# Attention scores of two heads at once, in plain fp32, in place of a split query times a split key

## The chip, the cores and the metric

The kernel runs on one core of one Trainium2 chip. The metric is the device time of the whole program in microseconds (us); a run's time is that of one launch.

## What is computed

Causal attention over a window of 128 keys plus 4 sink keys, then a mixture of experts with greedy assignment, then a dense feed-forward layer. Only the first step of the attention, the scores, is touched by the change:

```python
B, H, S, D = q.shape                        # 2, 8, 768, 64
scale = 1.0 / np.sqrt(D)
scores = scale * np.matmul(q, k.transpose(0, 1, 3, 2))
...
scores = np.where(keep, scores, -1000000000.0)   # 4 sinks, 128 keys back
scores = scores - np.max(scores, axis=-1, keepdims=True)
a = np.exp(scores)
a = a / (np.sum(a, axis=-1, keepdims=True) + 1e-09)
return np.matmul(a, v).astype(np.float32)
```

Its result `x`, 1536 tokens by 512, goes through `_moe_ref` (8 experts, 192 tokens each, 512 to 1024 to 512) and `_moe2_ref` (512 to 2048 to 512).

## The kernel before

The attention works on blocks of 128 queries. There are 2 batches times 6 blocks, so 12 steps (`STEPS`), and each step has 8 heads. For one head and one step the scores are a tile of 128 queries by 260 keys: the block's own 128 keys, the 128 before them, and 4 sinks.

The work is a pipeline by hand. Every engine runs `attention_slot(s)` for s = 0, 1, 2, and so on, and one slot holds pieces of three steps: the scores, the row maximum and the exponential of step s (`front`), the transposes of the probabilities, the sink terms and half of the products with v of step s - 1 (`mid`), and the rest of those products and the turn back to token rows with the gate's logits of step s - 2 (`end`). Slots 0 and 1 have nothing older to work on, and slots 12 and 13 have no scores. The order inside an engine is that of the loop over `h` in its `attention_slot`; between engines there are only semaphores.

**Scores before.** TensorE's fast fp32r form rounds its operands, so each operand is split in a rounded part and what is left. Host code hands q and k over twice, in partitions 0 to 63 and again in 64 to 127. `q_hl` holds the rounded q in the upper half of the rows and the rest in the lower half; `k_hi` and `k_lo` are the rounded k and its rest, in both halves. Two fp32r matmuls over all 128 rows (L1199), `q_hl` times `k_hi` and `q_hl` times `k_lo`, add up to the full product of one head in one of three PSUM banks (`S_BANK`). The split is made by other engines: ScalarE rounds k (L334, `round_next_k`), GpSimd rounds q (L328), and subtracts to get `k_lo` (L346) and the lower half of `q_hl` (L339). For the first two steps ScalarE and VectorE do parts of it.

**Around it.** `head_max` on VectorE (L817) reads a bank, applies the mask, writes the negated scores and their minimum, and so frees the bank. ScalarE's L642 is the exponential. `turn_prob` on TensorE (L1217) transposes a head's 128 by 256 probabilities in two instructions; a pair of heads fills a PSUM bank, which VectorE (L857, three of four pairs) or ScalarE (L662, one of four) copies to `prob_t`. `turn_sinks` (L1226), `sink_values` (L1237), `values` (L1253) and `turn_and_gate` (L1274) are the other matmuls of a slot. `values` writes one head to PSUM rows 0 to 63 and the next to rows 64 to 127, each through 64 columns of the array. `keep_clock` (L1174) multiplies zeros where TensorE would have nothing to do, 19 times before the first scores.

**Queues.** The SP queue loads q and k of step t + 2 in pass t of its loop, behind waits on `qk_split`, then stores a finished x block, then loads v. After the attention, later code sorts out routing (VectorE, L906) and runs experts and the feed-forward layer (L1409, L1418, L1500, L1511).

Of the kernel before, what the change touches and what calls it, by code (L numbers as in the profile page):

```python
# [17 lines left out]
F32 = mybir.dt.float32  # L18
# [11 lines left out]
P = 128  # L30
CAP = N // E
QB = S // P
# [25 lines left out]
def program(nc, q_t, k_t, k_sink, v_rows, v_sink_d, wg_d, w1_d, w2_d, w_in_d, w_out_d, alpha_d, out, n_sink, window):  # L58
# [9 lines left out]
    with ctx:  # L68
# [42 lines left out]
        q_raw = [sb(f"q_raw{b}", [P, H, P], at=early) for b in range(2)]  # L111
        k_raw = [sb(f"k_raw{b}", [P, H, P], at=early) for b in range(2)]
        ks_raw = sb("ks_raw", [P, B, H, NS], at=early)

        q_hl = [sb(f"q_hl{b}", [P, H, P], F32R, at=early) for b in range(2)]
        k_hi = [sb(f"k_hi{b}", [P, H, KW], F32R, at=early) for b in range(2)]
        k_lo = [sb(f"k_lo{b}", [P, H, KW], F32R, at=early) for b in range(2)]
# [78 lines left out]
        q_loaded = [sem(f"q_loaded{b}") for b in range(2)]  # L198
# [4 lines left out]
        q_hi_first = sem("q_hi_first")  # L203
        q_hi_done = sem("q_hi_done")
        k_hi_done = sem("k_hi_done")
        qk_split_first = sem("qk_split_first")
        qk_split = sem("qk_split")

        q_left_first, k_left_first = sem("q_left_first"), sem("k_left_first")
        k_lo_done = sem("k_lo_done")  # L210
# [111 lines left out]
        HEADS = (slice(0, H // 2), slice(H // 2, H))  # L322

        def round_q(eng, s, heads=slice(0, H)):

            b = s % 2
            copy = eng.tensor_copy if eng is nc.gpsimd else eng.copy
            return copy(q_hl[b][:, heads, :], q_raw[b][:, heads, :])  # L328

        def round_k(eng, s, heads=slice(0, H)):  # L330

            b, i = step(s)
            at = i % 2 * P
            return eng.copy(k_hi[b][:, heads, at:at + P], k_raw[b][:, heads, :])  # L334

        def rest_of_q(eng, s, heads=slice(0, H)):

            b = s % 2
            return eng.tensor_tensor(out=q_hl[b][D:P, heads, :], in0=q_raw[b][D:P, heads, :],  # L339
                                     in1=q_hl[b][D:P, heads, :].bitcast(F32), op=ALU.subtract)  # L340

        def rest_of_k(eng, s, heads=slice(0, H)):

            b, i = step(s)
            at = i % 2 * P
            return eng.tensor_tensor(out=k_lo[b][:, heads, at:at + P], in0=k_raw[b][:, heads, :],  # L346
                                     in1=k_hi[b][:, heads, at:at + P].bitcast(F32), op=ALU.subtract)
# [9 lines left out]
        def _(sp):  # L357
            def load_q(s):
                b, i = step(s)
                if s == 2:  # L360
                    sp.wait_ge(qk_split_first, 2)
                elif s > 2:
                    sp.wait_ge(qk_split, s - 2)
                sp.dma_start(q_raw[b][:, :, :], q_t[b, i, :, :].rearrange("d (h n) -> d h n", n=P)).then_inc(q_loaded[b], 16)

            def load_k(s):
                b, i = step(s)
                if s == 3:
                    sp.wait_ge(k_lo_done, 1)
                sp.dma_start(k_raw[b][:, :, :], k_t[b, i, :, :].rearrange("d (h n) -> d h n", n=P)).then_inc(k_loaded[b], 16)  # L370
# [22 lines left out]
            for n, heads in enumerate((slice(0, H // 2), slice(H // 2, H))):  # L393
                sp.dma_start(q_raw[0][:, heads, :], q_t[0, 0, :, :].rearrange("d (h n) -> d h n", n=P)[:, heads, :])\
                  .then_inc(q_first[n], 16)
            sp.wait_ge(k_first[0], 16)
            load_k(1)
            load_q(1)
            load_v(0)
# [1197 lines left out]
```

## Time and profile before

| what | value |
|---|---|
| median of 3 runs | 647.87 us (647.58 to 647.95) |
| the profiled execution's own time | 646.13 us |
| its span, first to last instruction | 644.4 us |
| TensorE matmul busy | 620.3 us, 96% of the span |
| VectorE, ScalarE, GpSimd busy | 65%, 47%, 30% |
| mean granted TensorE clock | 0.997 of 2.4 GHz |

The profiled execution is 1.7 us below the median of the runs. Its span leaves out 1.7 us before the first and after the last instruction. In the rows below PE is TensorE's matmuls, PEld its weight loads, DVE VectorE, ACT ScalarE, POOL GpSimd. The attention ends at about 112 us of the span; what follows is not touched by the change. A matmul of plain fp32 operands shows as two records, one of fp32r operands or a transpose as one.

### The profile page before, as it was taken

To read this page: it belongs to the slowest core of one execution; us is meant where nothing else is said; L and a number is where in the kernel's file an instruction comes from. 1 tells how busy PE (TensorE), PEld (TensorE's weight loads), DVE (VectorE), ACT (ScalarE), POOL (GpSimd) and SP (SyncE) were. 2 spreads that over 40 slices of the span, in tenths; PEclk is the share of its full clock that TensorE was granted. 3 is DMA by queue.
4 is the path that set the end of the run, shared out by engine and by line. 5 is a ranking of instruction groups with operands and counts; after the bars stand their busy time and mean duration, and the time that the engine had idled before them with its cause. 6 is when DMAs were issued, how large, how long until landed. Compare 5 with 4: busy or idle time off the path is not lost.

```text
span 644.4 us, 12853 instructions
## 1 busy us (share of the span) xinstructions
PE 620.3 (96%) x4926; PEld 554.2 (86%) x4933; DVE 418.6 (65%) x1148; ACT 299.7 (47%) x704; POOL 195.7 (30%) x212
## 2 busy tenths in 40 slices
PE   7899999989999999999999999999999999999994
PEld 4788897558899888899999888999988989999994
DVE  8688887988576979844759798438577520045551
ACT  5877784111122655532246554322566542346652
POOL 5988870010110342121113431201234420123322
PEclk9999999999999999999999999999999999999998
DMA  7477765525350143027103510470017610000001
GB/s 257 148 262 267 257 197 165 180 91 198 110 226 2 66 149 122 2 79 264 45 2 106 188 43 1 138 246 2 2 66 260 239 44 14 1 0 2 1 1 49
DMA packets 31284, 72.36 MB, mean 112 GB/s; under 512 B 2940, under 2 KB 3000, under 8 KB 31224
## 3 DMA queue, kind: packets, MB, share of 16 engines
q1 hardware_dynamic: 27232, 60.69, 27.3%
q0 software_dynamic: 2048, 6.29, 3.3%
q10 hardware_dynamic: 1944, 4.56, 2.0%
q8 instruction: 39, 0.64, 0.4%
q14 instruction: 21, 0.17, 0.1%
HBM read 65.22 MB, written 6.32 MB: 111 GB/s over the span
## 4 chain that ended last, share of the span: by engine, by line
PE 81%; DVE 5%; ACT 1%; issue 0%; POOL 0%; POOLq 0%; ACTq 0%; DVEq 0%
PE bank L1511 21%; PE bank L1500 20%; PE bank L1418 13%; PE bank L1409 13%; PE bank L1334 3%; DVE beats L906 3%; PE bank L1253 2%; PE bank L1217 1%; PE bank L1199 1%; PE bank L1387 1%; PE bank L1365 1%; PE bank L1274 1%; DVE ties L915 1%; PE bank L1349 0%; POOL out L603 0%
## 5 line engine op out<-in xcount | busy, mean ns | idle before, releaser
L580 POOL TENSOR_TENSOR wi_lo<-w_in,wi_hi 128x512 fp32r<-128x512 f32 x64 | 85.7, 1342 | 278.8 <-ACT wi_hi L706 278.8
L906 DVE TENSOR_SCALAR beats<-rank_row,key 128x512 bf16<-128x512 f32 (+11 forms) x173 | 105.7, 636 | 13.0 <-PE bank L1336 13.0
L1511 PE MATMUL bank<-wo_hi,g_lo 128*128 128x512 f32 x192 | 76.0, 396 | 0.0
L1511 PE MATMUL bank<-wo_lo,g_hi 128*128 128x512 f32 x192 | 75.8, 395 | 0.0
L1511 PE MATMUL bank<-wo_hi,g_hi 128*128 128x512 f32 x192 | 75.5, 393 | 0.0
L1156 DVE SCALAR_TENSOR_TENSOR g<-bank,g_neg 128x384 f32<-128x384 f32 x64 | 35.5, 555 | 57.4 <-ACT g_neg L760 57.1
L758 ACT ACTIVATE g_neg<-bank 128x384 f32<-128x384 f32 x64 | 31.4, 491 | 79.8 <-PE bank L1500 79.8
L1500 PE MATMUL bank<-y_hi,wi_hi 128*128 128x384 f32 x256 | 58.2, 349 | 1.3 <-DVE g L1156 1.3
L642 ACT ACTIVATE prob<-neg_s,neg_max 128x260 f32<-128x260 f32 x96 | 48.9, 510 | 18.7 <-DVE neg_max L817 17.3
L732 ACT ACTIVATE h_t<-bank 128x192 f32<-128x192 f32 x64 | 21.1, 330 | 74.1 <-PE bank L1409 74.1
L1500 PE MATMUL bank<-y_hi,wi_lo 128*128 128x384 f32 x256 | 55.3, 337 | 0.0
L1500 PE MATMUL bank<-y_lo,wi_hi 128*128 128x384 f32 x256 | 54.7, 334 | 0.0
L1146 DVE TENSOR_TENSOR g_lo<-g,g_hi 128x384 fp32r<-128x384 f32 x64 | 44.8, 700 | 14.7 <-ACT g_hi L765 14.5
L1024 DVE TENSOR_TENSOR y_lo<-bank,y_hi 128x192 fp32r<-128x192 f32 x32 | 11.3, 354 | 60.9 <-ACT y_hi L743 60.8
L1500 PEld LDWEIGHTS bank<-y_hi,wi_hi 128*128 128x128 f32 x256 | 44.2, 188 | 5.8 <-DVE g L1156 2.5
L1418 PE MATMUL bank<-h_t,w_b 128*128 128x192 f32 x256 | 47.7, 334 | 0.0
L1334 PEld LDWEIGHTS bank<-want,beats 128*128 128x128 bf16 x1008 | 34.1, 96 | 14.8 <-DVE beats L906 6.3
L915 DVE SCALAR_TENSOR_TENSOR ties<-rank_row,key,tri_after 128x128 bf16<-128x128 f32 x84 | 42.4, 505 | 6.4 <-DMA rank_row<-key_row 5.5
L743 ACT CAST y_hi<-bank 128x192 fp32r<-128x192 f32 x32 | 10.2, 319 | 77.5 <-PE bank L1418 77.5
L1500 PEld LDWEIGHTS bank<-y_hi,wi_lo 128*128 128x128 f32 x256 | 46.2, 188 | 0.0
L1409 PE MATMUL bank<-x_gt,w_b 128*128 128x192 f32 x256 | 45.3, 331 | 0.7 <-ACT x_gt L722 0.7
L1500 PEld LDWEIGHTS bank<-y_lo,wi_hi 128*128 128x128 f32 x256 | 45.3, 188 | 0.0
(163 smaller groups left out, 1340.7 us busy)
## 6 DMA issues: line engine op xcount, KB each, us to landing
w_a<-moe_w SPq DMA_DIRECT2D x8, 1024.0 KB, 5.1
w_a<-moe_w SPq DMA_DIRECT2D x4, 2048.0 KB, 10.2
w_b<-moe_w SPq DMA_DIRECT2D x8, 1024.0 KB, 5.1
w_b<-moe_w SPq DMA_DIRECT2D x4, 2048.0 KB, 10.3
k_raw<-k_t SPq DMA_DIRECT2D x11, 512.0 KB, 5.1
q_raw<-q_t SPq DMA_DIRECT2D x11, 512.0 KB, 3.7
w_in<-moe_w_in SPq DMA_DIRECT2D x8, 512.0 KB, 5.3
w_out<-moe_w_out SPq DMA_DIRECT2D x8, 512.0 KB, 5.6
```

The lines of the kernel that those rows point to most:

```text
L580: nc.gpsimd.tensor_tensor(out=wi_lo[:, f % 2, :, :], in0=w_in[:, :, f * P:(f + 1) * P], in1=wi_hi[:, f % 2, :, :].bitcast(F32), op=ALU.sub ...
L642: nc.scalar.activation(prob[b][:, h, :], neg_s[:, h % 4, :], ACT.Exp, bias=neg_max[b][:, h:h + 1], scale=-1.0, accum_out=p_sum[b][:, h, 0: ...
L758: nc.scalar.activation(g_neg[:, :], UP_BANK[f % 2][:, 0:GS], ACT.Relu, scale=-1.0).then_inc(neg_turned, 1)
L906: return nc.vector.tensor_scalar(out=beats[:, c % 3, lo:hi], in0=rank_row[:, lo:hi], scalar1=key[:, c:c + 1], scalar2=None, op0=op)
L915: nc.vector.scalar_tensor_tensor(out=ties[:, c % 3, :], in0=rank_row[:, c * P:(c + 1) * P], scalar=key[:, c:c + 1], in1=tri_after[:, :], o ...
L1146: nc.vector.tensor_tensor(out=g_lo[:, f % 3, :], in0=g[:, f % 2, :], in1=g_hi[:, f % 3, :].bitcast(F32), op=ALU.subtract).then_inc(g_split, 1)
L1156: nc.vector.scalar_tensor_tensor(out=g[:, f % 2, :], in0=u, scalar=0.0, in1=g_neg[:, :], op0=ALU.max, op1=ALU.add).then_inc(g_ready, 1)
L1334: nc.tensor.matmul(COUNTS[:, t, :], beats[:, c % 3, t * P:(t + 1) * P], want[:, c, :], start=False, stop=False, skip_group_check=True)
L1409: last = nc.tensor.matmul(into, w1[e][:, c, k * P:(k + 1) * P], x_gt[e][:, c, :], start=(c == 0), stop=(c == DC - 1))
L1418: last = nc.tensor.matmul(into, w2[e][:, f, m * P:(m + 1) * P], h_t[e][:, f, :], start=(f == 0), stop=(f == EC - 1))
L1500: last = nc.tensor.matmul(UP_BANK[f % 2][:, 0:GS], w[:, f % 2, c, :], y[:, c, :], start=(n == 0), stop=(n == len(passes) - 1))
L1511: last = nc.tensor.matmul(DOWN_BANK[t][:, :], a[:, f % 3, t * P:(t + 1) * P], w[:, f % 2, :], start=(f == 0 and n == 0), stop=(f == FC - 1 ...
```

## The change

The scores are now plain fp32 matmuls. The host packs a pair of heads: the first head's 64 dimensions in partitions 0 to 63, the second's in 64 to 127. `scores(s, r)` issues two matmuls for pair `r`, one in the upper 64 rows of the array and one in the lower 64, each to its own PSUM bank. q and k go from DRAM straight into `q_sb` (four buffers) and `k_sb` (two, each for two blocks); all the rounding and subtracting is gone. The loads have half the bytes. `S_BANK` still has three banks, so a pair now waits until `head_max` is through with the first head of the pair before. `head_max` waits for both heads of its pair. The fourth pair's copy to `prob_t` goes from VectorE to ScalarE, which now has two of four. Before the first scores there are 12 `keep_clock` matmuls instead of 19. SP waits for `scored` where it waited for `qk_split`.

```diff
-        q_raw = [sb(f"q_raw{b}", [P, H, P], at=early) for b in range(2)]
-        k_raw = [sb(f"k_raw{b}", [P, H, P], at=early) for b in range(2)]
-        q_hl = [sb(f"q_hl{b}", [P, H, P], F32R, at=early) for b in range(2)]
-        k_hi = [sb(f"k_hi{b}", [P, H, KW], F32R, at=early) for b in range(2)]
-        k_lo = [sb(f"k_lo{b}", [P, H, KW], F32R, at=early) for b in range(2)]
+        q_sb = [sb(f"q_sb{n}", [P, PAIRS, P], at=early) for n in range(4)]
+        k_sb = [sb(f"k_sb{b}", [P, PAIRS, KW], at=early) for b in range(2)]
...
             def load_q(s):
                 b, i = step(s)
-                if s == 2:
-                    sp.wait_ge(qk_split_first, 2)
-                elif s > 2:
-                    sp.wait_ge(qk_split, s - 2)
-                sp.dma_start(q_raw[b][:, :, :], q_t[b, i, :, :].rearrange("d (h n) -> d h n", n=P)).then_inc(q_loaded[b], 16)
+                if s >= 4:
+                    sp.wait_ge(scored, H * (s - 3))
+                sp.dma_start(q_sb[s % 4][:, :, :], q_t[b, i, :, :].rearrange("d (r n) -> d r n", n=P)).then_inc(q_loaded[s % 4], 16)
...
-                if s == 3:
-                    sp.wait_ge(k_lo_done, 1)
-                sp.dma_start(k_raw[b][:, :, :], k_t[b, i, :, :].rearrange("d (h n) -> d h n", n=P)).then_inc(k_loaded[b], 16)
+                if s >= 2:
+                    sp.wait_ge(scored, H * (s - 1))
+                at = i % 2 * P
+                sp.dma_start(k_sb[b][:, :, at:at + P], k_t[b, i, :, :].rearrange("d (r n) -> d r n", n=P)).then_inc(k_loaded[b], 16)
...
-                if nxt < STEPS:
-                    b, i = step(nxt)
-                    pool.wait_ge(q_loaded[b], 16 * (i + b))
-                    if nxt >= 2:
-                        pool.wait_ge(scored, H * (nxt - 1))
-                    round_q(nc.gpsimd, nxt).then_inc(q_hi_done, 1)
...
-                        rest_of_k(nc.gpsimd, nxt).then_inc(k_lo_done, 1)
...
-                        rest_of_q(nc.gpsimd, nxt).then_inc(qk_split, 1)
...
-                    if h == 0 and 1 < front + 1 < STEPS:
-                        round_next_k(front + 1)
...
-                    if h == 3 and 0 <= mid < STEPS:
-                        g = 4 * mid + 1
+                    if h in (3, 7) and 0 <= mid < STEPS:
+                        g = 4 * mid + h // 2
...
-                dve.wait_ge(scored, n + 1)
+                dve.wait_ge(scored, n // 2 * 2 + 2)
...
-                        if h in (1, 5, 7):
+                        if h in (1, 5):
...
-                if n >= 3:
-                    pe.wait_ge(maxed, n - 2)
-                for k in (k_hi, k_lo):
-                    last = nc.tensor.matmul(S_BANK[n % 3][:, 0:KW], q_hl[b][:, h, :], k[b][:, h, :],
-                                            start=(k is k_hi), stop=(k is k_lo))
-                last.then_inc(scored, 1)
+                if n >= 2:
+                    pe.wait_ge(maxed, n - 1)
+                for half in range(2):
+                    rows = slice(half * D, (half + 1) * D)
+                    nc.tensor.matmul(S_BANK[(n + half) % 3][:, 0:KW], q_sb[s % 4][rows, r, :], k_sb[b][rows, r, :],
+                                     start=True, stop=True).then_inc(scored, 1)
...
-                    if front < STEPS:
-                        scores(front, h)
+                    if front < STEPS and h % 2 == 0:
+                        scores(front, h // 2)
...
-            keep_clock(19, PT_BANK[0])
+            keep_clock(12, PT_BANK[0])
```

The order on TensorE around the border of two slots, before: the last `values` of slot s, then the scores of heads 0 and 1 of slot s + 1 with transposes between, `values` again, the sinks' transpose and heads 2 and 3.

```order
L1253 MATMUL bank<-prob_t,v_sb 64x128 x8
L1199 MATMUL bank<-k_hi,q_hl 128x260
L1199 MATMUL bank<-k_lo,q_hl 128x260
L1217 MATMUL bank<-ident,prob 128x128 x2
L1199 MATMUL bank<-k_hi,q_hl 128x260
L1199 MATMUL bank<-k_lo,q_hl 128x260
L1217 MATMUL bank<-ident,prob 128x128 x2
L1253 MATMUL bank<-prob_t,v_sb 64x128 x8
L1226 MATMUL bank<-ident,sink_p 96x128
L1199 MATMUL bank<-k_hi,q_hl 128x260
L1199 MATMUL bank<-k_lo,q_hl 128x260
L1217 MATMUL bank<-ident,prob 128x128 x2
```

The same place now (L1152 is `values`, L1102 the scores, L1119 the transposes, L1128 the sinks' transpose, L1173 `turn_and_gate`), and on to the third pair:

```order
L1152 MATMUL bank<-prob_t,v_sb 64x128 x8
L1102 MATMUL bank<-k_sb,q_sb 128x260 x2
L1119 MATMUL bank<-ident,prob 128x128 x4
L1152 MATMUL bank<-prob_t,v_sb 64x128 x8
L1128 MATMUL bank<-ident,sink_p 96x128
L1102 MATMUL bank<-k_sb,q_sb 128x260 x2
L1119 MATMUL bank<-ident,prob 128x128 x4
L1102 MATMUL bank<-k_sb,q_sb 128x260 x2
L1119 MATMUL bank<-ident,prob 128x128 x2
L1173 MATMUL bank<-turn_gate,o_t 128x144 x2
L1119 MATMUL bank<-ident,prob 128x128 x2
```

Scores come in twos with the transposes of two heads behind them. The second pair is followed by the third with four transposes between, and nothing else.

On GpSimd, the instructions between one packing of the sinks and the next, before:

```order
L508 COPY sink_p<-prob 128x32 x3
L328 CAST q_hl<-q_raw 128x1024
L346 TENSOR_TENSOR k_lo<-k_raw,k_hi 128x8x128
L339 TENSOR_TENSOR q_hl<-q_raw,q_hl 64x1024
L452 MEMSET mask_even 128x260
L447 AFFINE_SELECT mask_even<-mask_even 128x128 x3
```

And now:

```order
L474 TENSOR_TENSOR v_sink_parts<-v_sink,v_sink_parts 32x512
L415 MEMSET mask_even 128x260
L410 AFFINE_SELECT mask_even<-mask_even 128x128 x3
L468 COPY sink_p<-prob 128x32 x6
L415 MEMSET mask_odd 128x260
L410 AFFINE_SELECT mask_odd<-mask_odd 128x128 x3
```

The cast and the two subtractions of each step are gone from the engine; packing sinks and building masks are what is left on it.

## Rows read from the trace of the kernel before

**Rows 1.** Page, busy time by engine: us (share of the span) xinstructions.

```profile
PE 620.3 (96%) x4926; PEld 554.2 (86%) x4933; DVE 418.6 (65%) x1148; ACT 299.7 (47%) x704; POOL 195.7 (30%) x212
```

**Rows 2.** Stretches, one per slot: length, then PE, PEld, DVE, ACT, POOL busy.

```profile
31.50:39.80 8.30, 7.85 (x81) 6.96 (x77) 6.66 (x28) 6.46 (x21) 7.44 (x11) 1.00 0.76 256
72.10:79.70 7.60, 7.60 (x77) 6.96 (x77) 6.52 (x27) 6.28 (x20) 6.26 (x6) 1.00 0.80 275
```

**Rows 3.** Timeline, PE: first scores of slots 0, 1, 2, 11; first transpose of 12.

```profile
7.58 0.36 PE L1199 MATMUL bank<-k_hi,q_hl 128*128 128x260 f32 x1
...
13.48 0.36 PE L1199 MATMUL bank<-k_hi,q_hl 128*128 128x260 f32 x1
...
23.77 0.39 PE L1199 MATMUL bank<-k_hi,q_hl 128*128 128x260 f32 x1 [0.40 <-POOL q_hl L339]
...
95.03 0.39 PE L1199 MATMUL bank<-k_hi,q_hl 128*128 128x260 f32 x1
...
102.68 0.66 PE L1217 MATMUL bank<-ident,prob 128*128 128x128 f32 x4
```

**Rows 4.** Chain of waits, slot 9: start us, us on the chain, work xrecords.

```profile
81.96 0.24 PE bank L1226
...
83.60 0.49 PE bank L1274 x4
...
84.56 0.41 PE bank L1237 x4
...
85.97 0.25 PE bank L1199 x2
86.22 0.22 PE bank L1217 x2
86.44 1.02 PE bank L1253 x16
87.46 0.44 PE bank L1199 x2
```

**Rows 5.** Timeline, PE, behind a `values` group: start us, us.

```profile
87.39 0.39 PE L1199 MATMUL bank<-k_hi,q_hl 128*128 128x260 f32 x1
87.62 0.29 PE L1199 MATMUL bank<-k_lo,q_hl 128*128 128x260 f32 x1
87.74 0.38 PE L1217 MATMUL bank<-ident,prob 128*128 128x128 f32 x2
```

**Rows 6.** Timeline, PE, first and last records of one `values` group.

```profile
86.37 0.33 PE L1253 MATMUL bank<-prob_t,v_sb 128*64 128x128 f32 x2
...
87.18 0.28 PE L1253 MATMUL bank<-prob_t,v_sb 128*64 128x128 f32 x2
```

**Rows 7.** Timeline, PE: into a group of 64-row transposes and out of it.

```profile
146.93 0.27 PE L1387 MATMUL bank<-ident,x_g 128*128 128x128 f32 x1
...
147.13 0.27 PE L1387 MATMUL bank<-ident,x_g 64*128 64x64 f32 x1
...
147.37 0.22 PE L1387 MATMUL bank<-ident,x_g 64*128 64x64 f32 x1
147.52 0.18 PE L1334 MATMUL bank<-want,beats 128*128 128x9 bf16 x1
```

**Rows 8.** Timeline of the start, PEld and ACT.

```profile
5.29 0.62 ACT L334 CAST k_hi<-k_raw 128x512 fp32r<-128x512 f32 x1 [0.22 <-DMA k_raw<-k_t]
...
5.86 1.39 PEld L1174 LDWEIGHTS bank<-zeros 128*128 128x128 bf16 x7 [0.20 <-issue]
...
9.93 0.51 ACT L642 ACTIVATE prob<-neg_s,neg_max 128x260 f32<-128x260 f32 x1
```

**Rows 9.** Timeline, DVE: one head's maximum.

```profile
73.73 0.42 DVE L817 CUSTOM_DVE_ANT_0 neg_s<-bank,mask_even 128x260 f32<-128x260 f32 x1
74.08 0.08 DVE L817 DVE_READ_ACCUMULATOR2_ANT neg_max<- 128x1 f32 x1
```

**Rows 10.** Waits, 0 to 130 us: total us, times, longest.

```profile
PEld bank L1199 <- POOL q_hl L339: 3.4, 10, 0.6
```

## What I expect of the change, before seeing it run

> **What bounds the kernel now.** I read the page first. TensorE's matmuls are busy 96% of the span, no other engine over 65% [rows 1]. That is an average over stages, so next come the stretches of single slots. In slot 3 and in slot 8 PE is busy for all but a little of the slot, while DVE is busy 6.5 to 6.7 us, ACT 6.3 to 6.5 us and POOL 6.3 to 7.4 us of it [rows 2]. The chain of waits says the same: in slot 9 it runs through PE alone, one matmul line after the other, and the pieces join without a gap [rows 4]. So in a steady slot the price of every record on PE counts, and the splitting on POOL and ACT costs only where it is late.
>
> The timeline gives the slots' lengths [rows 3]. Slot 0 starts at 7.58 us, slot 1 at 13.48, slot 2 at 23.77, and slot 12, the first without scores, at 102.68. Slot 11 lasts 102.68 - 95.03 = 7.65 us; nothing waits there. Ten such slots would be 76.5 us, but slots 2 to 11 took 78.9. The 2.4 us between are PE waiting for POOL: slot 3 alone is 8.3 us long [rows 2], and the waits put 3.4 us of idle weight loading down to POOL's `q_hl`, in 10 waits [rows 10].
>
> **Removed.** Two heads' scores are four records in 2 x 0.245 = 0.49 us of chain (0.25 and 0.24 alternate from head to head); behind a `values` group the first head costs 0.44 [rows 4]. With POOL's three large operations a step gone, its lateness goes: 2.4 us. ACT loses a cast and gets a copy, DVE loses a copy, SP's loads halve in bytes. None of the three is on the path of a steady slot [rows 2, 4], so I count nothing; their cover is PE's own work, and it gets longer. SP now asks for k of step t + 2 when the scores of step t are through, with a whole slot to land in, and the store and the load of v behind it in the queue also have a slot.
>
> **Added, per pair of heads.** Four records of 260 columns, two for each half of the array. Four steps are priced by rows.
> - Streaming. Plain fp32 `turn_and_gate` has four records of 144 columns in 0.49 us of chain [rows 4], 0.85 ns a column, so 260 columns are 0.22 us. Do the halves overlap? No row shows two row halves at work. The bounds are 0.44 us for the pair, if they overlap fully, and 0.88 if not at all. The nearest rows are the `values`, which use two column halves: their records start in twos, at the group's head (two records in 0.33 us) as at its end (two in 0.28) [rows 6], and 16 records of 128 columns take 1.02 us [rows 4], where 0.11 each one by one would be 1.75. I take 0.44. Below that is nothing, since each half must stream its own two records.
> - The way in and out. Going from full-array transposes to 64-row ones, the next start comes 0.20 us later (146.93 to 147.13) against 0.11 of a plain transpose; on the way back it comes 0.15 later (147.37 to 147.52) against 0.06 [rows 7]. That is 0.09 each way.
> - The first weight load after a switch lies open: behind `values` the second score record starts 0.23 us after the first, and the next one 0.12 after that [rows 5], so 0.10 to 0.11 for 128 columns. The transposes behind the pair have the same, at 0.05 (the first 64-row step is 0.11 against 0.06 [rows 7]).
> - Sum: 0.09 + 0.10 + 0.44 + 0.09 + 0.05 = 0.77 us a pair, against 0.49. The new order has three such pairs in a slot; the fourth, at the slot's start, comes right behind `values`, where the way in and the load were paid before as well (0.44 + 0.245 = 0.68), so it adds only 0.09. A slot grows by 3 x 0.28 + 0.09 = 0.93 us.
>
> **The banks.** A pair now waits until the first maximum of the pair before is through. That is the load 0.10, streaming 0.44, 0.17 of tail (a record of 0.29 us whose successor starts after 0.12 [rows 5]) and 0.43 on DVE [rows 9], with hand-overs some 1.2 us. A pair with its four transposes (0.44 [rows 4]) takes 0.77 + 0.44 = 1.21. Between the second and third pair nothing else stands, so I add 0.04 us a slot there. Queued behind the wait is the whole of PE, but elsewhere `values`, `turn_and_gate` or the sinks fill the time. A steady slot is then 7.65 + 0.97 = 8.62 us.
>
> **The start.** The last seven `keep_clock` matmuls run from 5.86 us on at 0.2 us each [rows 8], and they go: the first scores move from 7.58 to about 6.1. Data is there, since k's first half had landed at 5.29 even with twice the bytes [rows 8]. Slot 0 is four rounds of pair, two `keep_clock` and bank wait, 1.25 us each: 5.0, against 5.9 now, ending at 11.2. Slot 1 has four rounds of 1.21, the sinks 0.24 + 0.41, `values` 1.02 and a way into it 0.1 [rows 4], and I add 0.5 for the chain from the last exponential over the sinks' packing: 7.1 us, against 10.3, in which POOL, DVE and ACT were still splitting (the first exponential ran at 9.93 [rows 8]). Slot 2 starts at 18.3 instead of 23.77: 5.5 us gained.
>
> **Sum.** 10 x 0.97 - 2.4 - 5.5 = +1.8 us. The profiled execution would go from 646.13 to 647.9. The median of the runs shown is 1.7 us above that execution, so I predict 649.7 us against 647.87.
>
> **Rivals.**
> - *No price for switching* (the one on the other side). If the 64-row halves are fed while the full array is still draining, a pair is 0.44 us plus nothing, and a slot's scores shrink: three pairs by 0.05 and the first by about as much. But the bank wait decides then: pair two to three would take 0.88 us and must take 1.15, so 0.27 comes back. A slot is 7.72, slots 0 and 1 end near 17.0, and the end of slot 11 is at 94.2 instead of 102.68: -8.5 us, 639.4. For it: the start gains anyway, and the point of balance is near, at 0.73 us a pair in place of 0.77. Against it: rows 7 show both ways paid in full, also to 64 rows. Partly true cases fill 640 to 646.5.
> - *The second half follows a pass behind.* The compiled order is first half twice, then second half twice. If the third record may start only with the second, a pair takes three passes, 0.22 us more, in 48 pairs +10.6: 660.3. Against it speak the twos at head and end of the `values` group [rows 6]. The Trainium skill, "TensorE: Matmul & The Clock Gate", Part 3, says matmuls keep strict program order in start and end, and by it this rival would hold; in this trace the column halves do not behave so, with 0.33 us for the first two records together. Whether row halves do, no row shows.
> - *No overlap of row halves*: 0.44 more per pair, 48 pairs, +21: 671.
> - *The two halves' weight loads follow each other*: 0.10 more per pair, +4.8: 654.5. In `values` they would be hidden by their 64 columns, so rows say little.
>
> **Numbers.** My forecast has 0.55, with 647 to 652.5 as its own range (0.02 us a pair is 1 us, the start is uncertain by 1.5). The rival without switching price, in full or part, has 0.20, the loads 0.10, the pass behind 0.10, no overlap 0.05. The range, 642.5 to 656.5, takes in the forecast, the loads and the upper half of the fast rival, and leaves out the last two and the rest. About 0.2% (1.3 us) is what a measurement of this kernel can tell from no change. Of my forecast's 0.55, 0.17 lies within that and 0.03 below it, so faster has 0.23, same 0.17 and slower 0.60.
>
> **What would show it.** Right: slots 2 to 10 of even length near 8.6 us, with no wait on POOL; the scores' records in twos, the second two 0.2 to 0.3 us after the first; 0.2 us from the last transpose to the first score and 0.3 from the last score to the next transpose; slot 2 starting near 18.3 us. Wrong: records of the lower half starting with the upper half's second or behind it; transposes starting right behind scores; PE idle on `neg_max` in most pairs; a slot length that ACT or DVE fills; or any change after the attention, which should last as long as before from slot 12 on.

## The result, and the profile after

The changed kernel takes 650.37 us in the median of 20 runs (648.05 to 652.28); the kernel before, run 20 times beside it, 647.57 us. The ratio is 1.0039, with a 95% interval of 1.0024 to 1.0055: slower by 2.5 us, with 1.6 to 3.6 as bounds (the two medians themselves differ by 2.8). The forecast was 649.7 us against 647.87, slower by 1.8.

The runs fall in two groups, ten from 648.05 to 648.9 us, whose mean granted clock is 0.997 or 0.998, and ten from 651.85 to 652.3, with 0.990 or 0.991. The median, 650.37, lies in the gap between them, where no run is. The execution that was profiled took 652.1 us and is one of the upper group. Its span is 650.4 us, 6.0 more than the 644.4 of before. Two places make up these 6.0 us, and neither is all of the median's difference.

The page first, the row that answers to [rows 1]: busy us by engine.

```profile
PE 632.3 (97%) x4919; PEld 545.9 (84%) x4926; DVE 405.7 (62%) x1127; ACT 295.0 (45%) x701; POOL 134.1 (21%) x178
```

GpSimd lost 62 us of work, TensorE gained 12. Next the slots, as in [rows 3]: first scores of slots 0, 1, 2 and 11, and the first transpose of slot 12.

```profile
6.50 0.90 PE L1102 MATMUL bank<-k_sb,q_sb 64*128 64x260 f32 x4
...
12.07 0.49 PE L1102 MATMUL bank<-k_sb,q_sb 64*128 64x260 f32 x2
...
19.54 0.71 PE L1102 MATMUL bank<-k_sb,q_sb 64*128 64x260 f32 x4
...
97.20 0.71 PE L1102 MATMUL bank<-k_sb,q_sb 64*128 64x260 f32 x4
...
105.83 0.66 PE L1119 MATMUL bank<-ident,prob 128*128 128x128 f32 x4
```

Nine slots from 19.54 to 97.20 take 77.66 us, 8.63 each, and every one of them is 8.63 within 0.01. Slot 2 starts 4.2 us earlier than before (23.77), slot 12 starts 3.15 later (102.68). Slots 2 to 11 took 86.3 us instead of 78.9: +7.4, less 4.2, is +3.15.

Two of these slots as stretches, to lay beside [rows 2]: PE is busy for all of the slot, DVE and ACT for 6.1 us of 8.63.

```profile
36.80:45.43 8.63, 8.63 (x80) 6.19 (x79) 6.09 (x26) 6.11 (x21) 1.65 (x8) 1.00 0.56 181
71.32:79.94 8.62, 8.62 (x79) 6.18 (x77) 6.10 (x26) 6.10 (x21) 0.51 (x4) 1.00 0.54 184
```

The chain of waits runs through PE alone, as in [rows 4], now with these pieces (start us, us, work):

```profile
81.24 1.02 PE bank L1152 x16
82.26 0.25 PE bank L1128
82.51 0.64 PE bank L1102 x4
83.15 0.59 PE bank L1119 x4
83.73 0.69 PE bank L1102 x4
84.42 0.37 PE bank L1119 x2
84.79 0.49 PE bank L1173 x4
85.28 0.22 PE bank L1119 x2
```

A pair of scores holds the chain for 0.64 us, and 0.69 in the one place where it also waits for a bank. Four transposes behind it take 0.59 instead of 0.44, two take 0.37 instead of 0.22. So a pair with what it adds to its transposes costs 0.64 + 0.15 = 0.79 us, against 0.49.

The other 2.8 us are lost behind the attention. Stretches of 1 us (the number behind POOL's is the granted clock), of the kernel after, then the same place of before:

```profile
149.00:150.00 1.00, 0.53 (x15) 0.54 (x16) 1.00 (x4) 0.00 (x0) 0.00 (x0) 1.00 0.70 57
150.00:151.00 1.00, 1.00 (x8) 0.70 (x6) 1.00 (x4) 0.41 (x1) 0.00 (x0) 0.64 0.59 213
151.00:152.00 1.00, 1.00 (x28) 0.97 (x28) 0.94 (x3) 0.51 (x2) 0.00 (x0) 0.50 1.04 408
...
156.00:157.00 1.00, 1.00 (x5) 1.00 (x4) 0.43 (x1) 0.00 (x0) 0.00 (x0) 0.50 1.02 369
157.00:158.00 1.00, 1.00 (x18) 0.94 (x17) 0.16 (x1) 0.33 (x1) 0.00 (x0) 0.95 1.05 395
```

```profile
146.20:156.80 10.60, 10.57 (x152) 10.04 (x153) 10.60 (x24) 2.18 (x6) 0.00 (x0) 1.00 0.85 299
```

From 150.3 to 157 us TensorE had 0.50 of its clock, the lower of its two levels (1.2 instead of 2.4 GHz). Shortly ahead of that, up to 149.47, it waited 1.36 us for the first `beats` of the routing. But before had the same wait, at 146.23, and kept its clock; the timeline of after and then of before:

```profile
149.47 0.46 PE L1233 MATMUL bank<-want,beats 128*128 128x9 bf16 x12 [1.36 <-DVE beats L811]
```

```profile
146.23 0.46 PE L1334 MATMUL bank<-want,beats 128*128 128x9 bf16 x12 [1.36 <-DVE beats L906]
```

### The profile page after: what moved, and what is told of

Read it like the earlier page. It is cut to its first block, busy times and chain, and to the rows that moved or that the text cites. A ratio compares the mean times of both kernels' runs of the same rounds, so it can differ in the third digit from the quotient of the medians.

```text
span 650.4 us, 12749 instructions
## 1 busy us (share of the span) xinstructions
PE 632.3 (97%) x4919; PEld 545.9 (84%) x4926; DVE 405.7 (62%) x1127; ACT 295.0 (45%) x701; POOL 134.1 (21%) x178
## 4 chain that ended last, share of the span: by engine, by line
PE 91%; DVE 5%; ACT 2%; issue 1%; POOL 0%; POOLq 0%; ACTq 0%; DVEq 0%
PE bank L1410 21%; PE bank L1399 20%; PE bank L1308 14%; PE bank L1317 13%; PE bank L1102 5%; PE bank L1119 4%; PE bank L1152 4%; PE bank L1233 3%; DVE beats L811 3%; PE bank L1173 2%; PE bank L1079 1%; PE bank L1286 1%; PE bank L1264 1%; PE bank L1139 1%; DVE ties L820 1%
## 5 line engine op out<-in xcount | busy, mean ns | idle before, releaser
L1308 PE MATMUL bank<-x_gt,w_a 128*128 128x192 f32 x256 | 47.2, 341 | 0.0
```

The source lines that it names most:

```text
L1308: last = nc.tensor.matmul(into, w1[e][:, c, k * P:(k + 1) * P], x_gt[e][:, c, :], start=(c == 0), stop=(c == DC - 1))
```

## The experiments

Twelve kernels ran, in four sets, each beside 23 or 29 runs of the kernel before on its own chip. Ratios are to those.

### The price of a pair: full rows, and one head at a time

**full_array.** The other head's half of q is filled with zeros by the host, so that each head's scores are a plain fp32 matmul over all 128 rows and nothing switches.

```diff
-                    rows = slice(half * D, (half + 1) * D)
-                    nc.tensor.matmul(S_BANK[(n + half) % 3][:, 0:KW], q_sb[s % 4][rows, r, :], k_sb[b][rows, r, :],
+                    nc.tensor.matmul(S_BANK[(n + half) % 3][:, 0:KW], q_sb[s % 4][:, 2 * r + half, :], k_sb[b][:, r, :],
```

> The changed kernel with plain fp32 scores over all 128 rows of the array: q comes zero-padded per head (twice the bytes of q), the maximum waits for its own head only, nothing else differs. No row halves, so no way in or out, and no overlap. Theory (a pair costs 0.09 in, 0.10 open load, 0.44 streaming, 0.09 out, 0.055 open load of the transposes, together 0.78 us): a pair is now 4 x 0.22 = 0.885, so three pairs grow by 0.10 each, the one behind the values, which still pays 0.19 for leaving them, by 0.30. A steady slot goes from 8.63 to 9.2 us and the whole to +6 us. Rival (the switch is free and the pair in the changed kernel is long for its bank wait or its semaphores): full streaming of both heads adds 0.44 a pair, a slot is 10.4 us, the whole +18 us. Rival (the halves did not really overlap): a slot stays at 8.6 or gets shorter.

Measured: 656.05 us (2 runs), ratio 1.0123 (1.0104 to 1.0142); steady slots are 9.18 us, as expected. By the ratios the whole is 8.0 us above the kernel before and 5.4 above the changed kernel; the expected +6 fits only the second. The chain of waits has, per pair between transposes and behind `values`:

```profile
86.79 0.88 PE bank L1102 x4
...
91.88 1.07 PE bank L1102 x4
92.95 0.44 PE bank L1119 x4
```

0.88 us is four times 260 columns at 0.22, and the four transposes are back at 0.44. With halves the pair and its transposes take 0.64 + 0.59 = 1.23 us instead of 0.88 + 0.44 = 1.32: of the 0.44 us that the overlap saves, switching leaves 0.09. Behind `values`, where the switch is paid either way, it is 1.23 instead of 1.07 + 0.44 = 1.51, so 0.28 is left. 3 x 0.09 + 0.28 = 0.55 us a slot, which is 9.18 - 8.63. Two small terms cancel in it: the 0.05 us of bank wait at the third pair with halves, and 0.05 at the fourth pair on full rows, which takes 0.93 behind the sinks' product.

**single_heads.** The halves are still used, but each head is issued alone, ahead of its own two transposes. Same work, twice the switches, no overlap.

```diff
-                for half in range(2):
-                    rows = slice(half * D, (half + 1) * D)
-                    nc.tensor.matmul(S_BANK[(n + half) % 3][:, 0:KW], q_sb[s % 4][rows, r, :], k_sb[b][rows, r, :],
-                                     start=True, stop=True).then_inc(scored, 1)
+                rows = slice(half * D, (half + 1) * D)
+                nc.tensor.matmul(S_BANK[n % 3][:, 0:KW], q_sb[s % 4][rows, r, :], k_sb[b][rows, r, :],
+                                 start=True, stop=True).then_inc(scored, 1)
...
-                    if front < STEPS and h % 2 == 0:
-                        scores(front, h // 2)
+                    if front < STEPS:
+                        scores(front, h)
```

> The changed kernel with the scores of each head issued at its own place, so a 64-row matmul stands alone between full-array transposes: twice the switches, no overlap of halves. Theory: every head costs what a pair costs, 0.78 us, so a slot grows by 4 x 0.78 - 0.04 to 11.7 us and the whole by 35 us or more. Rival (no price for switching): only the streaming doubles, 4 x 0.44, a slot is 10.4 us, the whole +20 us.

Measured: 684.57 us (2 runs), ratio 1.0563 (1.0542 to 1.0584), steady slots of 11.68 or 11.69 us. Chain of waits:

```profile
86.19 0.63 PE bank L1102 x2
86.82 0.37 PE bank L1119 x2
```

This is the plainest evidence that the halves overlap: one head alone, two records, holds the chain for 0.63 us, and two heads, four records, for 0.64. The second head is free. Both prices, on the way in and behind, are paid once per group of scores, whether it has one head or two.

### Fewer switches

**grouped.** From slot 2 on, the second pair goes right ahead of the first group of `values`, and the fourth right ahead of the second group. `values` pays a switch anyway, so 9 changes of the array's shape in a slot are left of 11.

```diff
-                    if front < STEPS and h % 2 == 0:
+                    if front < STEPS and h in ((0, 4) if mid > 0 else (0, 2, 4, 6)):
                         scores(front, h // 2)
...
+                    if h == 1 and front < STEPS and mid > 0:
+                        scores(front, 1)
...
+                    if h == 7 and front < STEPS and mid > 0:
+                        scores(front, 3)
```

> The changed kernel with two pairs of scores moved right ahead of a values group (pair 1 ahead of the first, pair 3 ahead of the second) from slot 2 on, so that the array changes its tiling 9 times a slot instead of 11; same matmuls, same banks. Theory (each change costs 0.09 us and an open load of 0.05 to 0.10): a slot goes from 8.63 to 8.35 us, the attention gets 2.3 to 2.8 us shorter. Rival (what costs is the fp32 streaming or the bank wait, which both stay): a slot stays at 8.6 us, or grows where pair 1 now comes 1.2 us behind pair 0.

Measured: 648.32 us (647.35 to 648.65), ratio 1.0003 (0.9994 to 1.0013). Steady slots are 8.35 us, three of them 8.45. The timeline around the fourth and the first pair:

```profile
92.44 0.38 PE L1119 MATMUL bank<-ident,prob 128*128 128x128 f32 x2
92.75 0.71 PE L1102 MATMUL bank<-k_sb,q_sb 64*128 64x260 f32 x4
93.39 1.09 PE L1152 MATMUL bank<-prob_t,v_sb 128*64 128x128 f32 x16
94.42 0.71 PE L1102 MATMUL bank<-k_sb,q_sb 64*128 64x260 f32 x4
```

`values` starts 0.64 us after the pair and takes its 1.03 us as ever: between these two nothing is added. What went are two ways from scores back to transposes, 0.15 us each in the chain (0.09 and 0.05 in the forecast), and 0.28 a slot is what they gave. By the ratios it is 2.3 us less than the changed kernel takes, and level with the kernel before. How much of the 2.3 us comes from the slots the times don't tell: the changed kernel's median holds the long loss of clock in half of its runs, the times of grouped lie where its lower group lies, and six of the twelve have a mean clock of 0.993, as the profiled one, whose clock fell for 3.4 us behind the attention.

### The start

**start_19.** 19 `keep_clock` matmuls ahead of the first scores, as before the change.

```diff
-            keep_clock(12, PT_BANK[0])
+            keep_clock(19, PT_BANK[0])
```

> The changed kernel with 19 zero matmuls ahead of the first scores, as before the change. Theory (a part of the gain at the start comes from these seven): the first scores start at 7.9 to 8.1 us in place of 6.5, all slots keep their lengths (8.63 from slot 2 on), slot 2 starts near 20.9, and the time is 1.2 to 1.5 us above the changed kernel. Rival (the clock is what the zeros buy: with more of them slots 0 and 1 run faster): the difference is under 0.7 us.

Measured: 651.82 us (4 runs), ratio 1.0051 (1.0037 to 1.0066). The difference to the changed kernel's ratio is 0.0012, 0.8 us, between the two theories and within both intervals: the times don't settle it. The profile does: the first scores start at 8.31 us, a little later than expected, slot 2 starts at 21.15 us in place of 19.54, and slot 12 at 107.44 in place of 105.83, with the slots unchanged. The seven matmuls' place is worth 1.6 us in these two executions.

A third execution shows why they don't compare exactly. more_zeros (below) has the same start as the changed kernel, yet its first scores ran at 5.36 us, not 6.50. Timeline, the zeros of more_zeros and of after, up to the first scores:

```profile
2.52 2.90 PE L1079 MATMUL bank<-zeros 128*128 128x512 bf16 x9
5.36 0.71 PE L1102 MATMUL bank<-k_sb,q_sb 64*128 64x260 f32 x4
```

```profile
2.53 4.04 PE L1079 MATMUL bank<-zeros 128*128 128x512 bf16 x9
6.50 0.68 PE L1102 MATMUL bank<-k_sb,q_sb 64*128 64x260 f32 x2
```

The same zeros took 1.1 us longer in one execution than in the other. In after each of the twelve takes about 0.43 us, in more_zeros only the first seven do, and the other five 0.22. In after even the first scores are still slow: the second two records start at 7.01, 0.51 us behind the first two, where 0.32 is usual.

### The dip of the clock behind the attention

**more_zeros** and **before_zeros.** The changed kernel, and the kernel before, each with 10 zero matmuls in place of 5 ahead of the routing's first count, so that TensorE waits 0.28 us for `beats` and not 1.36. The timeline of more_zeros:

```profile
148.12 0.46 PE L1233 MATMUL bank<-want,beats 128*128 128x9 bf16 x12 [0.28 <-DVE beats L811]
```

```diff
-            keep_clock(5, spare)
+            keep_clock(10, spare)
```

> The changed kernel with 10 instead of 5 zero matmuls ahead of the first count of routing round 1, where TensorE otherwise stands idle 1.4 us for VectorE's comparisons; scores untouched. Theory (half of the changed kernel's runs, those near 652 us, lose some 3.7 us to a TensorE clock at half rate for 6.8 us behind that idle stretch; the others are near 648.4): with the idle filled none falls, all runs are near 648.4 and the median is 1.5 to 2 us below the changed kernel's 650.4, or +0.8 us against the kernel before. Rival (the two groups of times come from somewhere else, such as DMA): both groups stay.

Measured: 649.07 us (648.13 to 650.11, 12 runs), ratio 1.0017 (1.0005 to 1.0028). The upper group is gone, and nine of the twelve runs have a mean clock of 0.996 or more; one has 0.993. The times spread more than expected, over 2 us, and the median is 1.1 us above the kernel before by the ratio, not 0.8.

> The kernel before, with one edit: 10 zero matmuls in place of 5 ahead of the first routing count, where TensorE waits for VectorE. Theory (the idle stretch there lets the clock fall in some executions, in this kernel too): its times come closer together than those of the kernel before (646.0 to 650.4 in the last sets), no run with a clock under 0.993, median 647.0 to 647.5, ratio 0.998 to 1.000. Rival (only the changed kernel loses its clock there): times and spread as those of the kernel before, ratio 1.000, or slower by the zeros themselves, 0.2 us.

Measured: 648.75 us (646.87 to 650.85, 12 runs) against 648.26, ratio 1.0016 (1.0004 to 1.0029): a miss. The times did not come together, and five of the twelve runs have a mean clock under 0.993, where none was expected. Its profiled execution had no dip, but another wait in its place, 1.34 us for ScalarE in the experts, which the other profiles don't have:

```profile
288.48 1.57 PE L1409 MATMUL bank<-x_gt,w_a 128*128 128x192 f32 x8 [1.34 <-ACT h_t L732]
```

**grouped_zeros.** Both edits, grouped and 10 zeros.

> The grouped kernel (two pairs of scores a slot right ahead of the groups of values) with 10 zero matmuls in place of 5 ahead of the first routing count. Theory: the two effects add, slots of 8.35 us and no times of the upper group: 646.8 to 648.0, median 647.4, ratio 0.998 to 1.000. Rival (grouped had no dips to lose): 648.3 to 649, the zeros cost 0.2 to 0.7 us and give nothing back.

Measured: 648.0 us (646.08 to 649.02, 12 runs), ratio 0.9991 (0.9977 to 1.0005), against 1.0003 for grouped. The difference is smaller than the intervals: the two effects did not visibly add.

Over all profiled executions the picture is clearer than from the times. A dip is here a stretch in which TensorE is granted 0.50 of its clock. From the start of slot 12 to the end of the span it takes 541.7 to 542.3 us where no dip and no stray wait falls in between, 543.2 to 543.8 with a dip of 3.4 us (five kernels), and 544.5 to 544.6 with one of 6.8 (after, full_array, mixed); before_zeros, with its stray wait and no dip, takes 543.3. With the wait of 1.36 us there was a dip in seven of nine kernels (not in before and in single_heads), with 0.28 us in one of five (mixed_3). That is one execution of each kernel; the mean clock of every run says more. The profiled executions with 0.993 or less had a dip ahead of the span's last 10 us, those with 0.996 or more had none. By this sign the filled wait helped the changed kernel, from ten of 20 runs at 0.993 or less to one of 12. In grouped it is six of 12 and in grouped_zeros still five. And the kernel before is not free of dips either: 45 of the 98 runs of it beside the experiments are at 0.993 or less, and so are five of the 12 of before_zeros. Filling the wait did nothing there that shows. The wait is not the whole cause, and what else is stays open.

### GpSimd's lateness in the kernel before

**b_late.** The routing's constants are built in slot 12, where GpSimd has nothing else, in place of slot 6.

```diff
-                if s == 6:
+                if s == STEPS:
                     routing_consts()
```

> The kernel before, with one edit: the constants for the routing are built on GpSimd in slot 12, where no scores are left, in place of slot 6. Theory (the split on GpSimd is late, and TensorE waits for it): slot 7 of the kernel before takes 8.7 us against 7.65 to 7.99 of its neighbours, because these constants delay the split for it; it falls to about 7.75, and the time by 1.0 us, ratio 0.998 to 0.999. The other slots of 7.75 to 8.3 stay. Rival (slot 7 is long for another reason): no change, ratio 1.000.

Measured: 648.45 us (645.03 to 649.59) against 648.26, ratio 0.9996 (0.9981 to 1.001). The timeline shows the gain, first scores of slots 7 and 8, of before and then of b_late:

```profile
63.36 0.39 PE L1199 MATMUL bank<-k_hi,q_hl 128*128 128x260 f32 x1
...
72.09 0.39 PE L1199 MATMUL bank<-k_hi,q_hl 128*128 128x260 f32 x1 [0.35 <-POOL q_hl L339]
```

```profile
63.30 0.39 PE L1199 MATMUL bank<-k_hi,q_hl 128*128 128x260 f32 x1
...
70.94 0.39 PE L1199 MATMUL bank<-k_hi,q_hl 128*128 128x260 f32 x1
```

Slot 7 falls from 8.73 to 7.64 us, and slot 12 starts 1.15 us earlier. The span didn't shrink, because this execution had a dip and before's had none. The median says neither theory nor rival: ten of the twelve runs of b_late have a mean clock of 0.993 or less. The two at 0.997 took 645.03 and 645.24 us, the two of the kernel before beside them at 0.997 took 646.66 and 646.71; that is 1.5 us in the theory's direction, from two runs each.

### Both ways in one kernel

If direct scores gain at the start and lose in each steady slot, a kernel that has each where it pays should beat both.

**mixed.** The kernel before, with steps 0 and 1 in direct pairs. Cut to its core (the loads and the order of the splitting follow from it):

```diff
+                if s < 2:
...
+                    for keys in range(2):
+                        for half in range(2):
+                            rows = slice(half * D, (half + 1) * D)
+                            k = ks_raw[rows, b, h + half, :] if keys else k_raw[s][rows, h + half, :]
+                            last = nc.tensor.matmul(S_BANK[(n + half) % 3][:, 2 * P if keys else 0:KW if keys else P],
+                                                    q_raw[1][rows, h + half, :] if s else q_pairs[rows, h // 2, :], k, start=True, stop=True,
+                                                    skip_group_check=True)
...
-                if s == 6:
+                if s == STEPS:
                     routing_consts()
```

> Both ways in one kernel: steps 0 and 1 take their scores in pairs as plain fp32 straight from what was loaded (without the block before, which they don't have: 128 and 4 columns), steps 2 to 11 by the split as in the kernel before, with the routing constants in slot 12. Theory (the change gains at the start and loses in each steady slot): slot 2 starts at 17.7 to 18.5 us in place of 23.8, slots 2 to 11 last 77 to 78 us together, none over 8.3, and the time is 640.5 to 642.5, ratio 0.989 to 0.992. Rival (the split for step 2, on GpSimd and VectorE in the short slot 1, is not ready): slot 2 starts with a wait for q_hl or k_lo of 1 us or more, and the time is 643 to 645.

Measured: 648.17 us (645.64 to 650.67), ratio 0.999 (0.9974 to 1.0006). Slot 2 starts at 23.78 us, as late as before. ScalarE's rounding of the k of step 2, at the head of slot 1, waited for its load, and the exponentials and a copy stood behind it. TensorE idled 2.87 us, and then it had half its clock (row of 20 to 30 us: mean 0.68; single stretches of 1 us from 20 to 26 us show 0.50). So neither theory nor rival: TensorE doesn't wait for `q_hl` or `k_lo` at the start of slot 2.

```profile
16.23 1.04 ACT L332 CAST k_hi<-k_raw 128x1024 fp32r<-128x1024 f32 x1 [1.24 <-DMA k_raw<-k_t]
...
19.39 0.88 PE L1218 MATMUL bank<-ident,prob 128*128 128x128 f32 x4 [2.87 <-ACT prob_t L665]
...
23.78 0.58 PE L1200 MATMUL bank<-k_hi,q_hl 128*128 128x260 f32 x1
```

```profile
20.00:30.00 10.00, 9.41 (x72) 8.23 (x70) 6.07 (x23) 6.36 (x21) 6.07 (x7) 0.68 0.47 164
```

**mixed_2** and **mixed_2_zeros.** Loads and rounding in another order than in mixed, some zeros in slot 1; the second also with 10 zeros behind the attention. Cut to two places, against mixed:

```diff
             load_q(1)
-            load_v(0)
+            load_k(2)
+            load_q(2)
...
-                    if h == 0 and 0 < front + 1 < STEPS:
+                    if h == (3 if front == 1 else 0) and 2 <= front + 1 < STEPS:
                         round_next_k(front + 1)
```

> The mixed kernel with its start repaired: k and q of step 2 are loaded ahead of v, ScalarE rounds the k of step 2 in the middle of slot 1 and that of step 1 at its end (they stood at the head of slots 0 and 1, and the exponentials behind them waited for the load), GpSimd subtracts for step 1 after step 2, VectorE takes half of the split for step 3 too, and zero matmuls fill TensorE's waits in slot 1. Theory (the mixed kernel lost its gain to an idle stretch at 16 to 19 us and to the slow clock behind it, granted 0.50 from 20 to 26 us): no stretch of 20 to 30 us under 0.9, slot 2 starts at 18.5 to 20.5 us in place of 23.78, slots 2 to 11 last about 78 us; span 640.5 to 642.5 without a dip of the clock at 146 to 153 us, 643.5 to 645.5 with one; the times in two groups like these, median 643 to 646, ratio 0.991 to 0.997. Rival (the split for step 2 sets the start of slot 2, whatever is loaded first): slot 2 starts over 21.5 us, time over 646.

Measured: 648.13 us (647.27 to 649.91), ratio 0.9996 (0.9982 to 1.0011). Slot 2 starts at 23.80: the rival's number, but not its cause. Now ScalarE waits 2.76 us for the sinks' v, which the new order loads later, and the clock is at 0.50 again from 20.1 us on, for 6.8 us; the timeline of mixed_2_zeros, where the same wait is 2.93:

```profile
14.46 0.62 ACT L678 CAST v_sink_parts<-v_sink 96x512 fp32r<-96x512 f32 x1 [2.93 <-DMA v_sink<-v_sink_d]
```

> The same kernel, and 10 zero matmuls in place of 5 ahead of the first routing count, at 146 us. Theory (behind the idle stretch there the clock falls in some executions): all times in one group, the lower one of mixed_2 plus up to 0.7 us for the zeros, no stretch of 140 to 160 us under 0.95; median 642.5 to 644, ratio 0.990 to 0.995. Rival (the dip doesn't hang on this stretch): two groups again, median as in mixed_2.

Measured: 647.19 us (646.23 to 648.53) against 648.41, ratio 0.9974 (0.9959 to 0.9989). It is the one kernel of the study that is faster than the kernel before, by 1.7 us (0.7 to 2.7). That is well above the expected 642.5 to 644. Its slot 2 starts at 23.15, with the clock at 0.50 from 18.2 us on, for 6.8 us, and its slot 12 at 102.82, no earlier than in the kernel before (102.68). So by its profile the attention gained nothing, and what remains is that no dip fell behind it.

**mixed_3.** Slot 1 mended once more: GpSimd rounds the k of step 1, the sinks' v is rounded later, eight more zero matmuls. Of the edit, two of the places with zeros:

```diff
-                            keep_clock(1, X_BANK[1])
+                            keep_clock(3 if h == 6 else 1, X_BANK[1])
...
                         values(mid, 0)
                         values(mid, 1)
+                        if mid == 0:
+                            keep_clock(3, X_BANK[1])
```

> mixed_2_zeros with its slot 1 mended: GpSimd rounds the k of step 1 in slot 0, the sinks' v is rounded in slots 1 and 2 in place of at the end of slot 0 (ScalarE waited 2.9 us for its load there), and 8 more zero matmuls stand where TensorE waited in slot 1 (1.6 and 1.5 us). Theory (the idle stretches of 1.5 us in slot 1 bring the slow clock behind them, granted 0.50 to 0.55 from 18 to 24 us, which eats what the start gains): no stretch of 10 to 30 us under 0.9, slot 2 starts at 19.3 to 20.8 us in place of 23.15, slots 2 to 11 last 78 to 79 us; median 643 to 645, ratio 0.992 to 0.995. Rival (the slow clock there costs nothing, since the split on GpSimd and ScalarE sets the end of slot 1): clock up, slot 2 at 22.5 us or later, median within 0.5 us of mixed_2_zeros.

Measured: 647.61 us (646.56 to 649.76), ratio 0.9994 (0.9978 to 1.0009), slot 2 at 24.34, later than in mixed_2_zeros, and the clock at 0.50 from 20.8 us on, for 3.4 us. The wait has only moved: VectorE's half of the split waits 2.23 us for GpSimd's rounded q, the sinks' subtraction is queued behind it, and TensorE waits 2.04 for that.

```profile
19.59 0.69 DVE L339 TENSOR_TENSOR q_hl<-q_raw,q_hl 64x512 fp32r<-64x512 f32 x1 [2.23 <-POOL q_hl L327]
20.29 0.28 DVE L866 TENSOR_TENSOR sink_t<-bank,sink_t 32x128 fp32r<-32x128 f32 x1
```

```profile
20.72 0.99 PE L1252 MATMUL bank<-sink_t,v_sink_parts 96*128 96x128 f32 x4 [2.04 <-DVE sink_t L866]
```

So direct scores in the first two steps alone don't give the start's gain: with the splitting for step 2 still to be done in slot 1, three orders of the loads and of the splitting started slot 2 at 23.2 to 24.3 us, where the changed kernel starts it at 19.54. Whether a fourth order is earlier stays open.

## Why the prediction was right, and where not

**The price of a pair: right.** 0.77 us was forecast from 0.09 + 0.10 + 0.44 + 0.09 + 0.05. The chain shows 0.64 for the pair and 0.15 more for its transposes, 0.79. The term that lay open, 0.44 for both halves together, is settled by single_heads (0.63 for one head, 0.64 for two) and full_array (0.88 without halves). The runs show the 0.20 ahead of the records and the 0.15 behind them as wholes, and not how each splits into the way and the weight load. Behind `values` a pair adds 0.64 - 0.68 + 0.15 = 0.11, where 0.09 was forecast. The rival without overlap and the one with the loads in a row are out. So is the second half a pass behind: the records of both halves start together, in twos, and the second two 0.32 us later. The first two of one pair, the second two, and the next transpose:

```profile
88.57 0.49 PE L1102 MATMUL bank<-k_sb,q_sb 64*128 64x260 f32 x2
...
88.90 0.39 PE L1102 MATMUL bank<-k_sb,q_sb 64*128 64x260 f32 x2
89.21 0.33 PE L1119 MATMUL bank<-ident,prob 128*128 128x128 f32 x1
```

The program issues the first half's matmul, two records, and then the second's. The records have no numbers, but `scored` is counted up by the last record of a matmul, and in the trace those are the two at 88.90; so the two at 88.57 are the first of each half. By strict program order (the Trainium skill, "TensorE: Matmul & The Clock Gate", Part 3) the second half's first record could not start ahead of the first half's second; here it starts 0.32 us ahead of it.

**No price for switching: out.** The last transpose's record starts at 83.46, the scores' first at 83.72 (with the bank wait in it), their second two at 84.04 and the next transpose at 84.36: 0.32 us, where 0.3 was forecast; and a slot is 8.63 us, not 7.72. In grouped two changes fewer took 0.28 us out of a slot.

**The banks: right.** 0.04 a slot was forecast; the third pair takes 0.69 where the others take 0.64.

**The steady slot: right.** 8.62 forecast, 8.63 measured. POOL's lateness went, as forecast: TensorE waits for it nowhere in slots 2 to 11, and b_late shows separately that 1.1 of the 2.4 us came from one set of constants. Together +7.4 us over ten slots, where 10 x 0.97 - 2.4 = 7.3 stood.

**The start: the mechanism right, the size off.** "Slot 2 starts at 18.3 instead of 23.77: 5.5 us gained" was 1.2 us too much in this execution. 0.4 of it is the first scores (6.50 for 6.1), 0.6 slot 0 (5.57 for 5.0) and 0.4 slot 1 (7.47 for 7.1), less 0.1 of rounding. The first scores came late because all twelve zeros ran at 0.43 us each in this execution; in before the step to 0.22 came after eleven, at 5.86 us, and the forecast counted from there. In slot 0 the term that was too small is the bank wait: rounds of 1.25 us were forecast, and they take 1.24 to 1.37. The first takes 1.59, 0.2 of it from the slow records of its pair. In slot 1 TensorE waits 0.71 us for the sinks, where 0.5 stood for the whole chain to them; the rest of the 0.4 stays open.

```profile
17.95 0.63 PE L1139 MATMUL bank<-sink_t,v_sink_parts 96*128 96x128 f32 x4 [0.71 <-DVE sink_t L768]
```

The first scores' time varies by itself, from 5.36 to 6.50 us in six executions with 12 zeros, so part of the 1.2 us belongs to the execution. Slot 12 starts at 105.83 us in after and at 104.49 in more_zeros, which is the same kernel up to there, and at 102.68 and 103.23 in before and before_zeros. So the attention alone costs 1.3 to 3.2 us by these four, and the forecast of +1.8 lies in that range.

**After the attention: wrong.** "Any change after the attention, which should last as long as before from slot 12 on" was named as a sign of error, and there was one of 2.8 us in the profiled execution: the clock fell. The lower group of times, 648.05 to 648.9, is 0.5 to 1.3 us above the median of before, and the upper one 4.3 to 4.7; half and half they make the median's +2.8. The forecast's +1.8 lies between the groups, and came close to the median in part by luck: it had no clock in it. The groups' middles are 3.7 us apart and the dip is worth 2.8 in the profiles; the other 0.9 no profile explains. more_zeros, without the upper group, has +1.1 us by its ratio (1.0017).

What stays open is why the changed kernel fell into a dip of 6.8 us in half of its runs. The wait ahead of it is as long as in the kernel before, and TensorE's work in the 42 us before that is the same, 405 records in 37.98 us. The kernel before loses clock too, in about half of the runs beside the experiments, so its median holds dips as well, and the difference of the medians is not free of them on either side.

## What to carry to other kernels

Two matmuls over half the rows each stream together, but the way in and the way out are paid per group and not per matmul: 0.2 us in here and 0.15 behind, against the 0.44 that the overlap saves. Put such groups where the array changes its shape anyway, and count the changes in a slot before writing the code. Where TensorE bounds the steady state, emptying GpSimd by a third (195.7 to 134.1 us) is worth the waits on it that go, 2.4 us here, and no more.

## What the hardware showed that I had not expected

- The clock granted to TensorE fell to half for 3 to 7 us in the middle of busy stretches, in some executions of a kernel and not in others, which moves the time by some 1.5 or 2.8 us. Behind the attention it came mostly behind a wait of 1.36 us, once behind one of 0.28 us. The kernel before shows it in its mean clock about as often as the changed one. On a kernel of 650 us this is as large as the effect that was to be measured.
- The first zeros of a launch take 0.43 us each and later ones 0.22, and when that changes differs from execution to execution: nine of them took 2.90 us in one execution and 4.04 in another, while the row of granted clock reads 1.00 in both. Whatever follows starts as much later.
- In mixed_3 VectorE did the first half of its split in 0.69 us and the second, of the same size, in 1.97, and GpSimd's subtraction beside it took 2.86 us where it takes 2.35 to 2.40 elsewhere. What of the two slowed the other no run here tells apart.
